# Moving transposes, a weight fold and filler matmuls in the order of an attention and two-layer kernel

## The reference

```python
def sm_attn(qq, kk, vv):
    s = scale * np.matmul(qq, kk.transpose(0, 1, 3, 2))
    s = s - np.max(s, axis=-1, keepdims=True)
    a = np.exp(s)
    a = a / (np.sum(a, axis=-1, keepdims=True) + 1e-09)
    return np.matmul(a, vv)
p_packed = sm_attn(p, k, v)              # p: 8 x 8 x 32 x 64, k, v: 8 x 8 x 576 x 64
out = sm_attn(q, p_packed, p_packed)     # q: 8 x 8 x 576 x 64

# x: 4608 x 512, the heads side by side
rms = np.sqrt(np.mean(x * x, axis=-1, keepdims=True) + 1e-06)
xn = x / rms * rms_g
g = xn @ w_gate                          # 512 x 1536
silu = g * (1.0 / (1.0 + np.exp(-g)))
x = silu * (xn @ w_val) @ w_out          # 1536 x 512

h = x @ w_in                             # 512 x 2048
g = np.maximum(h, 0.0) + alpha * np.minimum(h, 0.0)
return g @ w_out2                        # 2048 x 512
```

## Time and profile before

| | |
|---|---|
| median of 3 runs | 1544.66 us (1544.5 to 1545.04) |
| the profiled execution's own time | 1544.5 us |
| its span in the trace | 1542.7 us |
| PE busy | 1532.0 us, 99% |
| DVE busy | 704.6 us, 46% |
| ACT busy | 430.2 us, 28% |
| POOL busy | 194.7 us, 13% |

### The profile page before, as it was taken

One profiled execution on the slowest core, in us unless ns is written; L12 is line 12 of the kernel. 1 busy time (PEld: TensorE's weight loads), 2 busy tenths in 40 slices (PEclk: granted clock), 3 DMA queues, 4 the chain that ended last, 5 costly groups with the idle time before them and its releaser, 6 DMA issues.

```text
span 1542.7 us, 23601 instructions
## 1 busy us (share of the span) xinstructions
PE 1532.0 (99%) x9468; PEld 1267.1 (82%) x9468; DVE 704.6 (46%) x1193; ACT 430.2 (28%) x752; POOL 194.7 (13%) x185
## 2 busy tenths in 40 slices
PE   8999999999999999999999999999999999999999
PEld 4988888887878888798888888888888888888887
DVE  5764555555554555444343333333333333333333
ACT  4454453444444353422111111111111111111111
POOL 2800000000000000074162001020202001020000
PEclk9999999999999999999999999999999999999999
DMA  9312212110121210144300000010100000010000
GB/s 357 110 40 66 66 66 67 64 56 17 65 66 66 66 64 6 43 131 141 136 1 28 27 27 27 0 54 0 55 0 27 27 27 27 0 54 0 27 1 28
DMA packets 53563, 82.35 MB, mean 53 GB/s; under 512 B 16240, under 2 KB 25456, under 8 KB 53104
## 3 DMA queue, kind: packets, MB, share of 16 engines
q1 hardware_dynamic: 48448, 72.31, 14.0%
q10 hardware_dynamic: 5040, 8.98, 1.5%
HBM read 59.25 MB, written 22.02 MB: 53 GB/s over the span
## 4 chain that ended last, share of the span: by engine, by line
PE 98%; DVE 1%; ACT 0%; issue 0%; POOL 0%; DVEq 0%; POOLq 0%
PE psum L678 31%; PE psum L680 30%; PE psum L679 30%; PE psum L818 3%; PE psum L774 1%; PE psum L730 1%; PE psum L762 1%; PE psum L715 1%; PE psum L701 1%; PE psum L954 1%; PE psum L787 0%; DVE e L1293 0%; DVE an_lo L1365 0%; PE psum L756 0%; ACT a_sb L1027 0%
## 5 line engine op out<-in xcount | busy, mean ns | idle before, releaser
L1497 DVE TENSOR_TENSOR h_lo<-g,h_hi 128x512 fp32r<-128x512 f32 x144 | 104.8, 728 | 473.0 <-ACT h_hi L1199 473.0
L1199 ACT CAST h_hi<-g 128x512 fp32r<-128x512 f32 x144 | 89.4, 621 | 633.9 <-PE psum L680 600.4
L678 PE MATMUL psum<-an_hi,m_hi 128*128 128x288 f32 x768 | 236.5, 308 | 0.7 <-DVE an_lo L1365 0.6
L679 PE MATMUL psum<-an_hi,m_lo 128*128 128x288 f32 x768 | 225.9, 294 | 0.0
L680 PE MATMUL psum<-an_lo,m_hi 128*128 128x288 f32 x768 | 225.8, 294 | 0.0
L678 PE MATMUL psum<-h_hi,ow_hi 128*128 128x512 f32 (+2 forms) x480 | 184.7, 385 | 0.1
L680 PE MATMUL psum<-h_lo,ow_hi 128*128 128x512 f32 (+2 forms) x480 | 177.7, 370 | 0.0
L679 PE MATMUL psum<-h_hi,ow_lo 128*128 128x512 f32 (+2 forms) x480 | 177.6, 370 | 0.0
L678 PEld LDWEIGHTS psum<-an_hi,m_hi 128*128 128x128 f32 x768 | 144.1, 188 | 22.4 <-issue 13.3
L679 PEld LDWEIGHTS psum<-an_hi,m_lo 128*128 128x128 f32 x768 | 144.3, 188 | 5.0
L1453 DVE TENSOR_TENSOR act_sb<-act_sb,psum 128x288 f32<-128x288 f32 x168 | 75.8, 451 | 157.3 <-PE psum L680 129.5
(11 more groups left out here) (154 smaller groups left out, 2376.2 us busy)
## 6 DMA issues: line engine op xcount, KB each, us to landing
k_sb<-k_t SPq DMA_DIRECT2D x16, 576.0 KB, 5.2
q_sb<-q_t SPq DMA_DIRECT2D x8, 1152.0 KB, 6.1
xs_raw<-y_mid SPq DMA_DIRECT2D x9, 1024.0 KB, 5.2
out_t<-o_sb ACTq DMA_DIRECT2D x34, 256.0 KB, 2.0
v_sb<-v_s SPq DMA_DIRECT2D x8, 1024.0 KB, 6.2
gv_sb<-w_gv SPq DMA_DIRECT2D x4, 1536.0 KB, 19.2
w_raw_front<-w SPq DMA_DIRECT2D x10, 512.0 KB, 3.7
y_mid<-y_low SPq DMA_DIRECT2D x7, 512.0 KB, 2.8
```

What stands on the lines that cost most here:

```text
L678: nc.tensor.matmul(dst, w_hi, hi, start=start, stop=False)
L679: nc.tensor.matmul(dst, w_lo, hi, start=False, stop=False)
L1199: nc.scalar.copy(h2_hi[:, f % 2, :], g32[:, f % 2, :]).then_inc(g_hi_done, 1)
L1497: nc.vector.tensor_tensor(h2_lo[:, s, :], g32[:, s, :], h2_hi[:, s, :].bitcast(F32), ALU.subtract).then_inc(g_lo_done, 1)
```

## The change

Four things change in the orders; no step is added or taken out but fillers.

- In tiles, PE does `turn_a2` one block earlier: after the down piece of block 5, and no more after block 6.
- DVE follows: at block 5 `norm0` and `norm1` come ahead of `turn_a0`, and `turn_a2` comes ahead of block 6's product. `turn_s0` and `gram` at block 8 come after `h_lo`; in the wide tiles block 8 has no `h_lo`, and nothing moves there.
- In the prologue, PE does `fold0` ahead of `tokens1`, and `fold1` ahead of `mean0`.
- The fillers: two and not three ahead of `fold0`, four and not two ahead of `gram0`, two new ones ahead of `fold2`, and four and not three ahead of the tiles.

```diff
 PE_PLACES = {
     (0, "after", 0): ["scores"],
-    (0, "after", 5): ["turn_a01"], (0, "after", 6): ["turn_a2"], (0, "between", 6): ["packed"],
+    (0, "after", 5): ["turn_a01"], (0, "between", 5): ["turn_a2"], (0, "between", 6): ["packed"],
...
 DVE_PLACES = {
-    (0, "between", 5): ["turn_a0", "norm0", "norm1"], (0, "after", 6): ["turn_a2"],
+    (0, "between", 5): ["norm0", "norm1", "turn_a0"], (0, "within", 6): ["turn_a2"],
     (0, "within", 7): ["packed"],
-    (0, "after", 8): ["turn_s0", "gram"], (0, "after", 9): ["shift0"], (0, "between", 9): ["turn_s1"],
+    (0, "between", 8): ["turn_s0", "gram"], (0, "after", 9): ["shift0"], (0, "between", 9): ["turn_s1"],
...
-FILLERS = {"scores0": (5, EARLY_BANK), "turn_a01": (3, EARLY_BANK), "fold0": (3, LATE_BANK), "gram0": (2, EARLY_BANK),
-           "tiles": (3, LATE_BANK)}
+FILLERS = {"scores0": (5, EARLY_BANK), "turn_a01": (3, EARLY_BANK), "fold0": (2, LATE_BANK), "gram0": (4, EARLY_BANK),
+           "fold2": (2, LATE_BANK), "tiles": (4, LATE_BANK)}
...
-            for name in ("scores0", "scores1", "turn_a01", "turn_a2", "packed", "turn_packed", "tokens0", "tokens1", "fold0",
-                         "gram0", "mean0", "fold1", "fold2", "fold3"):
+            for name in ("scores0", "scores1", "turn_a01", "turn_a2", "packed", "turn_packed", "tokens0", "fold0", "tokens1",
+                         "gram0", "fold1", "mean0", "fold2", "fold3"):
```

## The result

The kernel after takes **1557.27 us** in the median of three runs (1555.06 to 1557.85) against 1544.66 before (1544.5 to 1545.04): a ratio of **1.0078**, 95% interval 1.0055 to 1.0101. It is slower by 0.8%. The forecast was 1555.1 with a range of 1551 to 1558; the narrower range that it gave for its own case was 1553 to 1557, and the time lies just above that. The profiled execution after took 1557.15 us, with a span of 1555.3; before it was 1542.7. The traces have 12.6 us more to explain, against 10.4 predicted.

The account below looks back on a forecast made before the run. The prediction took TensorE (PE), busy for 99% of the span, as the bound, though not in the prologue. Prologue 3.2, wide tiles 7.0, first tile 0.5 and -0.3 gave +10.4 on 1544.66, so 1555.1 us; range 1551 to 1558.

Parts of the forecast that it names:

- Prologue, +3.2 predicted: Prologue: fold0 waits for weights landing at 18.9 and holds tokens1; 3.8 - 0.7 + 0.1 = +3.2 us, bounds +2.4 to +4.1.
- the middle case: Prologue: PE's clock falls to half only after fold0's start, making VectorE 3.8 us late, between 3.1 and 4.6.
- The rival that the prologue costs nothing: Prologue: weights are there when PE asks, or VectorE's order has room; 1551.5 us, chance 0.08.
- the sum on the fillers: Prologue: four fillers ahead of the Gram product take at worst 3.2 us, ending by 25.0, under cover until 25.3.
- Wide tiles, 6 times 1.16 = +7.0 predicted: Six wide tiles: PE's fifth-chunk transposes wait 1.16 us each for VectorE's copy; +7.0 us, bounds 3.7 to 7.8.
- the half of the four small instructions: Wide tiles: two sums and reciprocals now ahead of VectorE's copy delay it by 0.51 us per tile.
- the half of asking early: Wide tiles: PE asks a block earlier, before the copy ends; 0.6 us each, 3.7 in all, if sums cost nothing.
- The rival that the wait is met in time: Wide tiles: the copy's release comes by 578.83, so the six stands vanish; 1547.6 us, chance 0.05.
- The clock in the tiles: Tiles: rival that PE's clock falls to half at each stand, 1.65 us each of six; 1565.0 us, chance 0.06.
- First tile, +0.5 - 0.3 predicted: First tile: the same wait for VectorE's copy costs +0.5 us (0 to 0.7); a later PE stand goes, -0.3.
- the exchange at block 8: First tile: score transpose and Gram masks behind h_lo cost nothing, hidden by VectorE's 1.32 us idle; 0.5 without it.
- the -0.3: First tile: PE's 0.3 us stand for VectorE (75.50 to 75.93) should go, shifted by 3.6 us against POOL.

Follow-up runs that it names:

- e12: Kernel after, with the first gate and value weight transfer cut from three chunks to two, then four, three and three: 1553.95 us, ratio 1.0054.
- e7: Kernel after, with only fold0 put behind tokens1 again; fold1's place and all fillers stay: 1554.91 us, ratio 1.0069.
- e2: Kernel before, with only the prologue's order and fillers changed, tables as before: 1547.9 us, ratio 1.0018.
- e8: Kernel after, with eight fillers ahead of fold0 and not two: 1557.01 us, ratio 1.0075.
- e3: Kernel after, with VectorE's copy (turn_a0) ahead of the sums and reciprocals (norm0, norm1) again: 1553.59 us, ratio 1.0053.
- e5: Kernel before, with only PE's turn_a2 one block earlier, VectorE's orders as before: 1549.73 us, ratio 1.0037.
- e6: Kernel before, with only VectorE's moves (block 5, turn_a2, block 8), PE's order as before: 1545.68 us, ratio 1.0007.
- e11: Kernel after, with POOL filling the split output weights with zeros instead of computing them, so the result is wrong: 1555.91 us, ratio 1.007.
- e1: Kernel before, with only the tiles' order tables changed (PE's and VectorE's moves), prologue as before: 1553.29 us, ratio 1.0052.
- e9: Kernel before, with three fillers added between tokens0 and tokens1: 1544.21 us, ratio 0.9993.
- e10: Kernel before, with one filler and not three ahead of fold0: 1544.39 us, ratio 0.9997.
- e4: Kernel after, with turn_s0 and gram ahead of block 8's h_lo in the first tile again: 1556.84 us, ratio 1.0076.

## Why the prediction was right, and which terms were mis-sized

The traces have 2.2 us more than the 10.4 of the sum. By its terms that is -0.1 in the prologue, +0.5 in the wide tiles, +2.2 in the first tile and -0.4 behind the tiles. The two large terms hold in size and cause; the small one is off by more than its own bounds, and only the width of the range kept the time inside.

**Prologue, +3.2 predicted, 3.09 measured.** The step held in each part: stand until the landing (2.69 named), second tokens 3.6 late, the 0.7 at the Gram product given back. The clock fell a little after fold0's start, the middle case. e12 shows the cause by itself (an earlier landing returns 2.8), e7 that it is fold0's place and not the fillers (-2.4). The rival that the prologue costs nothing is out by e2. The 3.1 do hang on when the weights land, and that differs between executions: 18.8 after, about 19.5 in e8, and about 20 in e3, whose fold started at 19.98. e2's span and medians bracket it at 3.4 to 3.9. (The 21.75 for the middle case in the sum on the fillers should be 21.55, from 17.75 and 3.8; nothing hangs on it.)

**Wide tiles, 6 times 1.16 = +7.0 predicted, 6 times 1.25 = 7.5 measured.** The term was right in its mechanism and in both its halves: the half of the four small instructions by e3 (3.6 us of waits gone), the half of asking early by e5. Of the 0.09 between them, 0.04 is release (0.14 where I took 0.1); the rest lies behind the stand. e6 shows that neither half of the edit is slow alone: DVE's order alone makes no stand, and PE's alone makes 0.74. The rival that the wait is met in time is out by the seven waits.

**The clock in the tiles.** Its rival is out: the clock is 1.00 in 590.50 to 592.00, 1.03 us of named idle time between transposes, and 1.00 behind it; in six microseconds around each of the other five stands it is 1.00 too. The Trainium skill, "TensorE: Matmul & The Clock Gate", Part 4 (PE-mode transpose), says that transposes do not count as PE activity for the clock gate in the way that matmuls do; if that was so here, this stand and the transposes around it were still too short to matter. No run here separates transposes from other work.

**First tile, +0.5 - 0.3 predicted, 2.4 measured: the failed step.** Two things in it failed.

First, I took `h_lo` of block 5 as long as before (0.56 us, released by ACT's cast). It took 1.40, because it fell on the start of a POOL subtraction and not on its end. That is the 0.9 us by which the stand exceeds 0.5. e11, in which POOL is idle at that time, has 0.46 us and a stand of 0.48. It does not take the prologue's 3 us to bring this about. In all five executions whose tiles start at 30.26 to 30.64 (before, e1, e5, e6, e9) this `h_lo` takes 0.56 to 0.83 us; in all eight that start at 30.95 or later with POOL's work unchanged (e12, e10, e7, after, e4, e8, e2, e3) it takes 1.39 to 1.41 and starts 0.19 to 0.21 behind a subtraction of POOL. So e12, whose tiles start only 0.3 later than before, has the long `h_lo` and the whole stand. In e10 and e2, which have the old places of `turn_a2`, the long `h_lo` is there too and PE does not stand: the price comes from both together. The Trainium skill has this contention as a rule: "SBUF — State Buffer", "Who interferes with whom", says that a DVE instruction with two SBUF inputs contends with a GpSimd instruction that reads SBUF, and not with one that only writes it. The Trainium skill, "SBUF — State Buffer", "Summary: rules for kernel authors", says that the second of the two to issue is fully blocked until the first finishes. The trace agrees in kind: 1.40 and 1.50 beside subtractions, 0.46 beside a fill (68.60 to 69.13, under 68.82). Of a full block until the other ends it shows an end 0.3 us behind POOL's, less than the 0.46 that the subtraction takes alone.

Second, I costed the exchange at block 8 at nothing, with DVE's 1.32 us of idle time as cover. The reader that counts is not the tokens matmul of the earlier trace rows: PE asks for the masks three matmuls earlier, ahead of block 9's last ones, at 71.4. And the cover was counted without a long `h_lo`, which now stands ahead of the masks (69.48 to 70.98). The stand is 0.84. This one does not hang on a shift. In all seven executions with the new order and POOL's work unchanged (after, e1, e3, e6, e7, e8, e12), with tile starts from 30.26 to 35.34, `h_lo` of block 8 starts 0.10 or 0.11 behind POOL's subtraction and takes 1.50 or 1.51; in the old order, where the transposes and masks go first, it takes 0.87 to 0.95. POOL's cast ahead of that subtraction is itself released by DVE (68.69), so POOL comes with the tile. The stand is 0.82 to 0.84 in six of the seven, and 1.22 in e6, where PE comes to it without an earlier stand.

The rows named make 0.5 + 0.9 + 0.84 - 0.3 = 1.9, with the -0.3 of the next paragraph. The 0.31 at 41.39 and the 0.12 at 92.43 bring it to 2.4. Neither has an experiment of its own, but the rows of all runs sort them. The first goes with the length of the tile's first `h_lo` (38.99 after, beside a POOL subtraction from 38.28 to 39.56): where that takes 0.46 to 0.70 us (before, e1, e5, e6, e9, e11) PE does not stand; with 0.89 to 0.93 (after, e2, e3, e4, e7) it stands 0.31 to 0.35, and with 1.16 to 1.51 (e8, e10, e12) 0.57 to 0.59. The way leads over DVE's product and ACT's cast, which wait for that `h_lo`, to ACT's copy of the scores, which ends at 41.24 and is the named releaser in e7, e8, e10 and e12. So it is the first failure once more, in another block. The 0.12 at 92.43 is in every run with the new order at block 8 and in none with the old one; what delays DVE there I did not trace.

**The -0.3.** The stand of the earlier trace rows is gone after, so the sum was right, but by another road than I gave. I said that a shift against POOL would remove it. Yet it is there, with 0.28 or 0.29, in e2 and e10, which start later, and in e4 (at 81.15). It is there in every run with the old order at block 8 (before, e2, e4, e5, e9, e10) and gone in every run with the new one (after, e1, e3, e6, e7, e8, e11, e12). So this is the gain of the exchange at block 8, whose stands come to 0.84 + 0.12 - 0.30 = 0.66 in the first tile. Undone in the kernel after (e4), the exchange gives back 0.3, with the small stands that come instead; made alone in the kernel before (e6), it costs 1.0.

**Left open.** The offset falls from 12.99 to 12.6 over the second half of the program; nothing that the change touches runs there. It falls by 0.2 to 0.3 in e3, e4, e8 and e10 too and not in e1, e5 and e6, and I have no cause. The kernel before has its runs in two clusters, near 1544.2 and 1545.4, and e9 has only the lower one: whether its fillers did that is not shown. No version here is shown to beat the kernel before.

## What to carry to other kernels

When an instruction is moved ahead on a queue that never idles, compare the time at which it will ask with the end of its supplier's last step, in the order of time of both engines; if the supplier comes later, everything queued behind it pays the difference in every iteration, and moving small work ahead of the supplier adds its whole length. Before calling a neighbour's exchange free, find the first instruction that waits for the result, not the one that uses it. And a shift of a few tenths of a microsecond can change which operations of VectorE and GpSimd fall together: an operation with two SBUF inputs should not stand directly ahead of what the bounding engine waits for, while GpSimd is reading.

## What the runs showed of the hardware

- The same VectorE subtraction (128x288, two SBUF inputs) took 0.46 us with POOL idle or filling, and 1.40 and 1.50 us when a POOL subtraction of 1.29 to 1.30 us had started 0.1 to 0.2 us before it; it ended about 0.3 us after POOL's both times. Met nearer its end it took less: 0.56 in before (51.89, POOL's ends at 52.13) and 0.83 in e1 (51.88, POOL's ends at 52.40), again with its end 0.3 us behind.
- The landing of the first weights came 2.5 us earlier with 1024 KB for 1536, in one execution of e12; in the others 1536 KB landed between 18.5 and about 20. 0.5 MB at the 400 to 410 GB/s of these stretches is 1.3 us. Where the other 1.2 come from is open; I had expected 0.9 to 1.3 and got 2.8 at the tiles' start, some of which is the full clock that this execution kept.
- The same stand does not always drop the clock. The idle 1.47 us in the prologue before were followed by half clock in the profiled executions of before and e7, and not in those of e1, e5, e6 and e10, where PE's order up to there is the same. The stand of about 2.5 to 3.6 us at the weights was followed by half clock in all five that have it, after, e2, e3, e4 and e11, and one of 0.98 in e10 was followed by it as well. Stands of 1.7 to 1.95 us before the Gram product in e3, e8, e11 and e12 were not (1.00 behind them). So here the length of a stand does not tell whether the clock falls.
